# Agent attention into a ReLU-mixed MLP: query softmax one chunk further ahead, its weights transposed by DMA instead of TensorE

## What is computed

```python
a2k = sm(agents, k)          # 49 x 12480, softmax of scale * a @ b.T
agent_v = a2k @ v            # 49 x 128
q2a = sm(q, agents)          # 12480 x 49
x = q2a @ agent_v            # 12480 x 128, both batches: 24960 rows
h = x @ w_in                 # 24960 x 2048
g = np.maximum(h, 0.0) + alpha * np.minimum(h, 0.0)
out = g @ w_out              # 24960 x 128
```

## Time and profile before

| | |
|---|---|
| median of 3 runs | 944.57 us (943.56 to 944.73) |
| profiled execution, its own time | 944.28 us |
| span of its profile, first to last instruction | 942.8 us |
| mean granted TensorE clock | 0.991 |
| PE busy | 925.7 us (98%) |
| DVE, ACT, POOL busy | 635.4 (67%), 540.4 (57%), 109.1 us (12%) |
| DMA | 58.55 MB, 62 GB/s on average |

### The profile page before, as it was taken

One profiled execution on the slowest core, in us unless ns is written; L12 is line 12 of the kernel. 1 busy time (PEld: TensorE's weight loads), 2 busy tenths in 40 slices (PEclk: granted clock), 3 DMA queues, 4 the chain that ended last, 5 costly groups with the idle time before them and its releaser, 6 DMA issues.

```text
span 942.8 us, 16143 instructions
## 1 busy us (share of the span) xinstructions
PE 925.7 (98%) x5850; PEld 499.9 (53%) x5850; DVE 635.4 (67%) x926; ACT 540.4 (57%) x746; POOL 109.1 (12%) x142
## 2 busy tenths in 40 slices
PE   7899999999999999999999999999999999999998
PEld 7784555555546556554444444444444444444443
DVE  4567666666767767767776676766666666666664
ACT  2236565565565565565656666666666666656564
POOL 6220100101001001001001010101010101010101
PEclk9799999999999999999999999999999999999999
DMA  8650221221212311201101110101111110101010
GB/s 296 262 189 28 62 77 51 77 64 48 80 63 70 102 62 66 72 29 46 29 26 47 29 46 29 46 29 45 30 43 32 36 39 32 42 26 47 26 37 24
DMA packets 29922, 58.55 MB, mean 62 GB/s; under 512 B 5248, under 2 KB 24000, under 8 KB 29632
## 3 DMA queue, kind: packets, MB, share of 16 engines
q1 hardware_dynamic: 29600, 58.03, 18.9%
q10 hardware_dynamic: 288, 0.06, 0.0%
HBM read 40.49 MB, written 12.78 MB: 57 GB/s over the span
## 4 chain that ended last, share of the span: by engine, by line
PE 94%; DVE 2%; issue 2%; DMA 1%; ACT 1%; SPq 0%; POOLq 0%; ACTq 0%
PE ps L541 54%; PE ps L524 17%; PE ps L531 7%; PE ps L501 3%; PE ps L551 2%; PE ps L388 2%; PE ps L694 2%; PE ps L688 1%; PE ps L517 1%; PE ps L464 1%; DMA kv_s<-kT 1%; PE ps L412 1%; PE ps L482 1%; DVE r_lo L1105 0%; PE ps L419 0%
## 5 line engine op out<-in xcount | busy, mean ns | idle before, releaser
L1105 DVE SCALAR_TENSOR_TENSOR r_lo<-ps,r_hi 128x960 f16<-128x960 f32 x416 | 466.5, 1153 | 259.4 <-ACT r_hi L862 256.7
L862 ACT ACTIVATE r_hi<-ps 128x960 f16<-128x960 f32 x416 | 386.3, 967 | 154.3 <-PE ps L531 149.2
L541 PE MATMUL ps<-r_hi,w_hi 128*128 128x480 f16 x832 | 252.1, 369 | 0.3 <-DVE M_a L1057 0.3
L541 PE MATMUL ps<-r_hi,w_lo 128*128 128x480 f16 x832 | 248.1, 366 | 0.0
L541 PE MATMUL ps<-r_lo,w_hi 128*128 128x480 f16 x832 | 240.7, 366 | 0.0
L524 PE MATMUL ps<-PT,M_a 128*128 128x480 f16 x832 | 204.0, 366 | 0.7 <-DVE r_lo L1105 0.7
L373 POOL TENSOR_TENSOR y<-y_relu,y_lin 128x480 f32<-128x480 f32 x52 | 62.4, 1200 | 627.4 <-issue 377.3
L541 PEld LDWEIGHTS ps<-r_hi,w_lo 128*128 128x128 f16 x832 | 91.4, 111 | 68.5
L541 PEld LDWEIGHTS ps<-r_lo,w_hi 128*128 128x128 f16 x832 | 85.4, 106 | 71.0
L541 PEld LDWEIGHTS ps<-r_hi,w_hi 128*128 128x128 f16 x832 | 77.1, 106 | 86.0 <-issue 41.9
L524 PEld LDWEIGHTS ps<-PT,M_a 128*128 128x128 f16 x832 | 75.6, 98 | 80.1 <-DVE r_lo L1105 16.8
(11 more groups left out here) (146 smaller groups left out, 599.6 us busy)
## 6 DMA issues: line engine op xcount, KB each, us to landing
q_s<-qT SPq DMA_DIRECT2D x52, 240.0 KB, 2.6
out<-y SPq DMA_DIRECT2D x52, 240.0 KB, 2.0
kv_s<-kT SPq DMA_DIRECT2D x24, 512.0 KB, 4.4
kv_s<-vP SPq DMA_DIRECT2D x12, 512.0 KB, 6.7
kv_s<-vS SPq DMA_DIRECT2D x8, 768.0 KB, 4.4
PR<-PT SPq DMA_DIRECT2D x156, 30.0 KB, 1.9
w_lin<-w_out SPq DMA_DIRECT2D x1, 1024.0 KB, 6.8
w_inT_s<-w_inT SPq DMA_DIRECT2D x1, 1024.0 KB, 5.6
```

Source lines behind the costliest of these rows:

```text
L541: mm = pe.matmul(ps[:, OUT, 0:CHUNK], w[:, 2 * p + u, :], r[:, s, u, :], start=(p == 0 and u == 0 and k == 0), stop=(p == PAIRS - 1 and u ...
L862: act.activation(r_hi[:, p % RING, :, :], ps[:, at:at + 2, 0:CHUNK], ACT.Relu).then_inc(hi_ready, 1)
L1105: dve.scalar_tensor_tensor(out=r_lo[:, p % RING, :, :], in0=ps[:, at:at + 2, 0:CHUNK], scalar=0.0, in1=r_hi[:, p % RING, :, :], op0=ALU.ma ...
```

## The change

The softmax of chunk n + 2 now runs during chunk n; the scores of chunk n + 3 stand between the matmuls of second layer 6. `query_turn` and `query_out` are gone, with the float16 identity matrix. In their place SP issues four DMA transposes from `stack` into `PT`, waits for them, and then issues the three `PR` DMAs:

```diff
-            def spread(n, half):
-                sp.wait_ge(q_ready, n + 1)
+            def turn(n, half, read=None):
+                groups = QUADS * n - QUADS
+                ...
+                sp.wait_ge(stack_zero, 1)
+                if read is not None:
+                    sp.wait_ge(h_ready, groups)
+                sp.wait_ge(q_hi, n + 1)
+                sp.wait_ge(q_dup, n + 1)
+                sp.wait_ge(q_lo, n + 1)
+                for t in range(4):
+                    sp.dma_start(PT[:, half, t * WIDE:(t + 1) * WIDE], stack[:, t, :], transpose=True).then_inc(q_turned, 16)
+                sp.wait_ge(q_turned, 64 * n + 64)
                 for g in range(32, 128, 32):
                     sp.dma_start(PR[g:g + 32, half, :], PT[0:32, half, :]).then_inc(q_spread, 16)
...
-                    if not (last and half == 1):
-                        spread(n + 1, 1 - half)
+                    if there(n + 2):
+                        turn(n + 2, half, n)
```

`h_ready` at 4n + 4 (for n the chunk that is running) means that the running chunk has read its `PT` and `PR` for the last time, after its rest 3. `stack` stays a single buffer, now of 128 partitions (`WIDE`), zeroed once by DVE; ACT may write it for the next chunk only when the transposes of the one before have landed:

```diff
             def query_hi(n):
                 act.wait_ge(q_normed, n + 1)
-                act.activation(stack[:, :, 0:A], q_p[:, :, :], ACT.Copy).then_inc(q_hi, 1)
+                if not (isinstance(n, int) and n == 0):
+                    act.wait_ge(q_turned, 64 * n)
+                act.activation(stack[0:T, :, 0:A], q_p[:, :, :], ACT.Copy).then_inc(q_hi, 1)
```

`PT` and `PR` now have 4 groups of 128 columns of which 120 are used, so the matmuls that read them take four stretches of 120 columns:

```diff
+            def tokens(x, half):
+                return x[:, half, :].rearrange("p (t n) -> p t n", n=WIDE)[:, :, 0:T]
...
-                    pe.matmul(ps[:, 2 * slot(p) + u, 0:CHUNK], M_a[:, b, f:f + 128], PT[:, half, :],
+                    pe.matmul(by_tile(ps[:, 2 * slot(p) + u, 0:CHUNK]), M_a[:, b, f:f + 128], tokens(PT, half),
                               start=True, stop=False)
```

In PE's body the transposes and the waits in front of them leave, and the wait for `q_turned` comes ahead of the next chunk's tiles 0:

```diff
                     linear(half, b)
-                    if ahead:
-                        ...
-                        query_turn(n + 1)
                     pe.wait_ge(lo_ready, g + 5)
                     tiles(6, half, b)
...
+                        pe.wait_ge(q_turned, 64 * n + 128)
                         tiles(0, 1 - half, nb)
```

More of the change, by code:

```diff
@@ L373, in finish, with body @@
                 pool.tensor_tensor(y[:, half, :], y_relu[:, half, :], y_lin[:, half, :], ALU.add).then_inc(y_ready, 1)
-            def body(i, b, kind, last):
+            def body(i, b, kind):
                 for half in range(2):
                     n = 2 * i + half
-                    if not (last and half == 1):
-                        query_again(n + 1)
+                    if there(n + 2):
+                        query_again(n + 2)
                     finish(n, half, i)
@@ L508, in query_scores, with by_tile @@
                 mm.then_inc(q_scored, 1)
[L510 to L518, removed]
+            def tokens(x, half):
+                return x[:, half, :].rearrange("p (t n) -> p t n", n=WIDE)[:, :, 0:T]
+            def by_tile(x):
+                return x.rearrange("p (t n) -> p t n", n=T)
             def tiles(p, half, b):
@@ L550, in linear @@
                 for w, end in ((L_a, False), (L_b, True)):
-                    mm = pe.matmul(ps[:, 2 * LIN_SLOT, 0:CHUNK], w[:, b, :], PT[:, half, :], start=not end, stop=end)
+                    mm = pe.matmul(by_tile(ps[:, 2 * LIN_SLOT, 0:CHUNK]), w[:, b, :], tokens(PT, half), start=not end,
+                                   stop=end)
                 mm.then_inc(lin_ready, 1)
@@ L641, in body @@
                     nb = 1 if kind == MIX_REST and half == 1 else b
-                    nb2 = 1 if kind == MIX_REST else b
-                    ahead = not (last and half == 1)
+                    nb3 = 1 if kind == MIX_REST or kind == MIX and half == 1 else b
                     start = isinstance(n, int) and n == 0
@@ L902, in body @@
                     quad = 2 * QUADS * i + QUADS * half
-                    ahead = not (last and half == 1)
                     start = isinstance(n, int) and n == 0
                     relu_hi(g + 2, quad + 1, 2, start)
-                    if ahead:
-                        query_exp(n + 1)
+                    if there(n + 2):
+                        query_exp(n + 2)
                     relu_hi(g + 3, quad + 1, 3, start)
-                    if ahead:
-                        query_hi(n + 1)
+                    if there(n + 2):
+                        query_hi(n + 2)
                     if kind == KEYS or kind == TOP and half == 0:
@@ L919, in body @@
                     relu_hi(g + 5, quad + 2, 5, False)
-                    if ahead:
-                        query_out(n + 1, 1 - half)
                     act.wait_ge(lin_ready, n + 1)
@@ L1187, in body @@
                     g = 2 * PAIRS * i + PAIRS * half
-                    ahead = not (last and half == 1)
-                    if ahead and not (isinstance(n, int) and n == 0):
-                        query_shift(n + 1)
+                    if there(n + 2) and not (isinstance(n, int) and n == 0):
+                        query_shift(n + 2)
                     if kind == VALUES:
@@ L1214, in body @@
                         rest_low(1, SMALL)
-                    if ahead:
-                        query_lo(n + 1)
+                    if there(n + 2):
+                        query_lo(n + 2)
                     relu_lo(g + 4, 4)
@@ L1250, in body @@
                         linear_low(1)
-                    if ahead:
+                    if there(n + 1):
                         relu_lo(g + 8, 0)
```

214 lines of the change are left out of this document (110 added, 104 removed).

## The result

The kernel after takes 945.66 us (median of 20 runs, 943.64 to 948.92), the kernel before 944.21 (941.80 to 945.61) beside it: ratio 1.0018, 95% interval 1.0010 to 1.0026, that is 0.9 to 2.5 us slower. Forecast were 945.4 us and no measurable change, with 0.2% as what can be told from none: the measured 0.18% is inside that, though the interval leaves out a ratio of 1 and its upper end, 0.26%, is above it. The profiled execution took 946.44 us with a span of 944.3 and a mean granted clock of 0.991, as before.

A forecast was written before the change was run, and what follows sets the result against it. PE was taken to bound the kernel, level with the ACT and DVE chain; 944.28 - 0.85 + 1.1 + 0.7 - 0.6 = 944.6, with half a microsecond for risks 945.1, plus 0.29 for the median 945.4 us; range 939 to 951.

The forecast's parts named there:

- (a): Transposes off PE in loop chunks: the ACT and DVE chain is level with PE's work, so 34 chunks gain nothing.
- The rival of the full gain: PE gets its 0.21 us in full in each of 52 chunks: 934.6 us; chance 0.12.
- (b): Written-out chunks: 0.05 us gained in each of 14, 0.14 in chunks 48 and 49; together -0.85 us.
- (f): Scores of chunk 2 moved ahead in the first part: +0.7 us; chunk 49 without scores between its matmuls: -0.6 us.
- (c): ACT loses its copy into PT between pairs 5 and 6: it delays no pair, so nothing is gained.
- (d): New wait of `query_hi` on the previous chunk's DMA transposes: 11.3 us are available, 4 to 5 needed, so it fits.
- T: Time the four DMA transposes of a chunk take: 4 to 5 us, with bounds of 3.7 and 11.2.
- The third rival: `query_hi` waits for the transposes in every chunk if T is over 11.3, costing (T - 11.3) x 50; chance 0.05.
- (e): First part: DVE's sum ahead of `denominators` comes 2.1 us later, of which net +1.1 us remains.
- (i): Clock in the first part: PE's idle time grows to some 2.6 us; a second slow stretch would cost 1.7, not summed.
- (g): SP's queue in the first part: batch 1's key piece behind the transposes; free up to T = 5.3, so nothing.
- (h): Four stretches of 120 columns in 34 matmuls a chunk: column count unchanged, so nothing.

The follow-up runs named there:

- the kernel before with k = 1: Kernel before with one matmul of second layer 4 moved from behind rest 3 to between tiles 6 and tiles 7: 942.80 us, 0.9988.
- the kernel after with its first part changed: Kernel after with chunk 2's scores ahead of the denominators and DVE's division of chunk 1 and shift of chunk 2 later: 944.28 us, 1.0003 of before.

## Why the prediction was right, and where it was not

*Loops, (a).* Right: stretch 4.31, period 15.88, the wait grown by 0.20. The rival of the full gain is shown wrong by the run with one transpose, which has neither the DMA nor the moved first part and gains nothing either.

*Written-out chunks, (b), and chunk 49, end of (f).* Forecast -0.85 and -0.6, together -1.45; the profile has -1.75 over the chunks and -0.22 in the end. Chunks 48 and 49 gain 0.08 each and the others 0.05 each, as forecast. What (a) left out with "nothing is won elsewhere" is chunk 8: there PE waited 0.20 us for the `PR` copies in the kernel before, and rest 3 to the next rest 0 falls from 3.93 to 3.66, since these copies now come a chunk ahead. The end is not chunk work: from SP's issue of the last store to the end of the span it is 2.63 us before and 2.41 after, 2.6 to 2.7 in every profile with the transposes on PE and 2.4 to 2.5 in every one with DMA transposes.

*ACT, (c).* Nothing, as forecast: `relu_hi` of pair 4 starts at rest 2 plus 0.51, as before and not under 0.43.

*The transposes, (d).* T was mis-sized: 6.1 us, not 4 to 5. An issue of a transpose takes SP 1.23 us and not the copies' 0.6, and it lands after 2.4 us and not 1.9: 3 x 1.23 + 2.4 = 6.1. It lay within the bounds, and the window of 11.3 us holds it. One rest later still fits (6.1 + 3.7 = 9.8 us), two do not (6.1 + 3.7 + 4.25 = 14.0). The third rival's place came out as it said, and its price, T less 11.3, in the last loop (2.7); in the longer chunks ahead of it the price was lower, and the rival left out the clock, which adds some 1.7 in two chunks of three.

*DVE in the first part, (e).* From the first keys to the 16 matmuls behind `denominators` it is 28.92 us before and 30.01 after: 1.09, forecast 1.1. The wait of PE there is 2.29, which 1.25 plus the step's 1.1 gives; (i) had written 2.6 for it.

*The key piece, (g).* Its result, nothing, is right, but two of its terms are wrong and offset each other. The step said free up to T = 5.3, and the prediction named T over 5.3 as a sign of being wrong; T is 6.2. The other is the start. The step let the transposes begin at 57.5, where POOL ended its shifts in the kernel before, but POOL had waited 6.82 us for ACT in the midst of them, for the very `query_again(0)` that the change moves. In the kernel after the shifts end at 51.24, `stack` is complete at 52.82 (DVE's low parts), and what holds the transposes until 56.95 is SP's own queue, the values and chunk 2's queries ahead of them. The 0.98 of the first keys taken off, they begin at 55.97, 1.5 us sooner than the step had it. So the key piece (issued at 66.62) landed at 70.59, or 69.61, where the step wanted it at 69.6, and PE took it at 70.78: there were 0.2 us to spare. With that little slack it is a limit of its own right behind (e): with (e) undone, the key piece came no sooner.

*Scores of chunk 2, (f).* The term that was furthest off, 0.7 forecast: from the key piece to the first second layer it is 9.56 us before and 10.79 after, 1.23. I gave PE 0.33 of cover from DVE's M_a. The first second layer carries scores of keys and waits for `q_shifted`, that is, for DVE's `query_shift(2)`, and this stands behind the very scores I had moved: the wait is now 0.75 for DVE's q_e (0.76 in the second profile of the kernel after). No cover, but a longer wait.

*Split rows, (h).* Nothing: L_b at 648.86, the next group at 649.06, 0.20 apart, as for unsplit ones.

*Clock, (i).* Windows of 4 us, before and then after, against the earlier trace rows:

```profile
68.00:72.00 4.00, 4.00 (x23) 3.17 (x22) 1.84 (x9) 0.74 (x2) 0.00 (x0) 0.84 0.42 151
```
```profile
64.00:68.00 4.00, 1.71 (x26) 1.43 (x24) 3.32 (x7) 0.00 (x0) 0.00 (x0) 0.97 0.32 72
68.00:72.00 4.00, 4.00 (x29) 3.50 (x25) 1.56 (x7) 0.89 (x3) 0.40 (x1) 0.61 0.96 365
```

Lost are 4 x (0.26 + 0.16) = 1.7 us before and 4 x (0.03 + 0.39) = 1.7 after: one stretch at 1.2 GHz in each, moved and not doubled. The half microsecond that I had set aside for (g) and (i) was not needed as such. The first part's clock is not fixed, though: the kernel before with k = 1 and the kernel after with its first part changed have no such stretch from 56 to 82 us in their profiles.

*The sum.* The span net of the first keys grew by 2.53 - 1.75 - 0.22 = 0.56 us, where the terms had 0.35 (1.1 + 0.7 - 0.6 - 0.85). A further 0.6 lies outside the span, which no step had: I took what lies around the span as fixed (0.29 to the median). It stood in for the half microsecond of risk, so the total of 945.4 was right by some luck in its parts. The 0.6 goes with the DMA transposes: it is in every kernel that has them and in none of the three changed kernels that keep them on PE. Those kernels also share the rest of the change, so the transposes are not shown to be its cause. What it is was not tried.

## What to carry to other kernels

When an engine holds the chain that ended last, ask at the place of a saving whether a second chain is level with it: here a 0.3 us wait of the weight loads, and the one chunk that lacked the work, told before the change that 0.21 us of PE a chunk would buy nothing. The saving was not lost but turned into a wait, and a matmul that does not depend on the awaited pair, put into it, won 10 us. Work moved ahead in a start-up phase should be priced behind every wait in it, in order: removing one (for DVE's sum) only uncovered the next ones, for SP's loads and for DVE's `av_rows`, and with the loads early the one for `av_rows` was left. A gain of 1 to 2 us there can also be the clock's, so look at the granted clock of both profiles before calling it the edit's.

## What the hardware showed that I had not expected

- A DMA transpose of a 128 x 128 fp16 tile costs SP 1.23 us to issue against 0.59 for a `PR` copy of as many bytes. Four are 6.1 us, of which the issues of the first three make 3.7. They also raise the packet count: the page has 63205 packets, 38528 of them under 512 B, where the kernel before has 29922 and 5248.
- With the transposes two rests late, the granted clock fell to 1.2 GHz behind 2.1 us without work of PE in 19 of the 22 chunks of the last loop, and cost up to 1.7 us each time, more than half of what the wait itself cost. In the other three chunks the same wait left it at 2.4 GHz.
- The same first part ran wholly at 2.4 GHz from 56 us on in one kernel's profile and had a stretch at 1.2 GHz in both profiles of another, which cost 1.4 us.
- Kernels with the DMA transposes take 0.6 us more outside the traced span (2.1 for 1.5), and 0.2 less from the last store's issue to its end.
